# Second products of the experts' scores on halves of the array, one set of masks, turned sums by transposes

## The chip, the cores and the metric

One core of one Trainium2 chip runs the whole program. The metric is the device time in microseconds, the median of repeated executions. Each execution does the same work on the same data.

## The reference, cut to what matters

Three layers follow each other, for 2 batches of 768 tokens. Everything is in f32, and the kernel keeps near f32 precision by splitting numbers into a high and a low part.

```python
# attention, 8 heads of 64: local window of 16 on each side, and block sums
scores_l = scale * q @ k.T                       # masked to |i - j| < 16
scores_s = scale * q @ k_max.T + log(32)         # k_max: maxima over 24 blocks of 32 keys
a = softmax(concatenate([scores_l, scores_s]))
x = a @ concatenate([v, v_mean])                 # v_mean: means over the 24 blocks
# four experts with causal attention of one head of 64, top 2 of 4 by a gate
for e in range(4):
    s = scale * (x @ wq[e]) @ (x @ wk[e]).T      # masked above the diagonal
    out += weight[e] * softmax(s) @ (x @ wv[e]) @ wo[e]
# token mixing (768 -> 256 -> 768) and channel mixing (512 -> 1536 -> 512)
u = out + (relu(out.T @ w_tok1) @ w_tok2).T
result = u + relu(u @ w_ch1) @ w_ch2
```

## The kernel before, in words

The five engines run written-out programs and meet through semaphores. The order of instructions on each engine is fixed by hand: `sequence(b, more)` exists once for TensorE (PE), ScalarE (ACT) and VectorE (DVE), and GpSimd (POOL) and SyncE have loops of their own. Both batches pass through attention, experts and token mixing one after the other. Channel mixing (from about 228 us on) then takes both batches and half of the time; the change doesn't touch it.

**Attention.** A unit is a tile of 128 queries of four heads, 12 units a batch (`NU`). `a_scores(b, u)` (L774) writes the scores of a unit into one of two PSUM pairs of banks `ps_s`. A unit has 4 x 120 columns: 96 keys of a window and 24 block maxima for each head. Every product there is 64 rows by 64 columns of the array, so four go on its quarters. It first writes a mask: `ident_b` (bf16 identity) times `mask_m` (0 or -1e9 in the window, the rounded log(32) in the 24 columns behind it), 4 products of 240 columns. Then 4 products `mask_w` times `mask_c`, 48 columns each, add what rounding took from log(32). Then come 8 products of queries and keys `QT`, `KW` in f32, each of them two passes on PE. DVE takes the maxima (`a_maxima`), ACT the exponentials (`a_exps`), POOL normalises, PE turns the weights (`a_transpose`, L841) and multiplies by the values (`a_values`).

`means(out, b, q)` (L816) turns the block sums of the values, `vsum`, so that blocks lie on partitions 96 to 119: two f32 products with the identity for each call, on 24 columns of the array, two calls a batch. In batch 1 the first call stands between products of token mixing of batch 0. ACT scales the result and spreads it over the value windows (`a_means`).

**Experts.** Queries and keys of expert e are stored so that one product gives two: `QS` holds the high part of the queries on the expert's own 64 partitions and the low part on the other 64; `KH` holds the high part of the keys on both. `KL` holds the low part of the keys on the own half, and zeros on the other, which POOL writes once a batch (`no_lows`, L659; PE waits for it by `m_kz` before unit 0). So a score tile is QS x KH + QS x KL, both over 128 rows, and a bf16 product `ident_b` x `causal` adds the mask to the 128 columns on the diagonal.

`UNITS` (L112) lists 14 units a batch as (query tile t, experts, stride of their columns in PSUM): tiles 0 and 1 have one unit with all four experts, tiles 2 and 3 two units with two, tiles 4 and 5 four units with one. An expert of tile t has (t + 1) x 128 columns, in pieces of at most 512. `m_scores(b, u)` (L910) goes through the experts and for each through KH, KL, and mask (in tile 0 one 512-column mask comes first instead). Then DVE takes maxima (`m_maxima`), ACT exponentials into `PM` (`m_exps`), PE turns blocks of 128 (`m_transpose`, L947), DVE and ACT copy the two PSUM banks of `ps_t` to `PTM` (`m_to_sbuf`, one on each), PE multiplies by the values `VE` (`m_values`, on 64 columns of the array each, two experts at a time).

PE's order in the experts' loop at step k is: scores of unit k, transposes of unit k - 2, output projection and spreading of weights where due, values of unit k - 3. Scores of unit u wait for the exponentials of unit u - 2, since `ps_s` has two buffers.

The projections, the experts' scores and both mixings use the format fp32r, where a product has one record in the trace; plain f32 products (attention's keys and values, the experts' values, the turned sums) have two. L764 is the helper `mm`, so in the profile nearly every product has that line and goes by its tiles.

## Time and profile before

| | us |
|---|---|
| median of 3 timed executions | 439.59 (439.43 to 439.99) |
| profiled execution, its time | 439.09 |
| its span, first to last instruction | 437.1 |
| PE busy | 426.0 |
| VectorE busy | 288.8 |
| ScalarE busy | 227.3 |
| GpSimd busy | 143.1 |

The profiled execution is the one that all rows below come from. Its own time is 0.5 us under the median; 2.0 us of it lie outside the span. A matmul's record has the start, which is exact, and an end that is modelled and covers its way through the array; successive ones overlap, so the distance of two starts is what one costs the engine. Records with the same names are merged in the timeline ("x16"), with the start of the first and the time to the end of the last. TensorE's granted clock is at its full level in the whole span.

### The profile page before, as it was taken

To read this page: it belongs to the slowest core of one execution; us is meant where nothing else is said; L and a number is where in the kernel's file an instruction comes from. 1 tells how busy PE (TensorE), PEld (TensorE's weight loads), DVE (VectorE), ACT (ScalarE), POOL (GpSimd) and SP (SyncE) were. 2 spreads that over 40 slices of the span, in tenths; PEclk is the share of its full clock that TensorE was granted. 3 is DMA by queue.
4 is the path that set the end of the run, shared out by engine and by line. 5 is a ranking of instruction groups with operands and counts; after the bars stand their busy time and mean duration, and the time that the engine had idled before them with its cause. 6 is when DMAs were issued, how large, how long until landed. Compare 5 with 4: busy or idle time off the path is not lost.

```text
span 437.1 us, 8551 instructions
## 1 busy us (share of the span) xinstructions
PE 426.0 (97%) x3326; PEld 364.0 (83%) x3326; DVE 288.8 (66%) x520; ACT 227.3 (52%) x581; POOL 143.1 (33%) x162
## 2 busy tenths in 40 slices
PE   6899999999999999999999999999999999999996
PEld 3679996887767899878877998898898889889985
DVE  4974569785478535776867875876765765565353
ACT  6895567774269836876846353443443233324120
POOL 4997927000039420002194465233122022200000
PEclk9999999999999999999999999999999999999999
DMA  8964370000870500000133013113113252301103
GB/s 294 346 214 139 110 288 0 1 2 1 304 287 8 170 1 2 0 1 1 25 113 105 1 49 96 49 48 97 50 48 96 81 178 78 97 0 49 48 0 145
DMA packets 14799, 39.66 MB, mean 91 GB/s; under 512 B 1656, under 2 KB 3368, under 8 KB 14760
## 3 DMA queue, kind: packets, MB, share of 16 engines
q1 hardware_dynamic: 14328, 38.60, 26.5%
q8 instruction: 27, 0.44, 0.4%
q10 hardware_dynamic: 432, 0.52, 0.3%
q14 instruction: 12, 0.10, 0.1%
HBM read 33.56 MB, written 4.72 MB: 88 GB/s over the span
## 4 chain that ended last, share of the span: by engine, by line
PE 90%; DVE 4%; POOL 3%; DMA 1%; issue 1%; SPq 0%; DVEq 0%
PE ps_s L764 36%; PE ps_o L764 20%; PE ps_x L764 16%; PE ps_t L764 11%; PE ps_t L947 4%; DMA QT<-in_qT 1%; POOL PA L606 1%; DVE vsum L1636 1%; PE ps_t L841 1%; DVE nmaxA L1471 1%; PE ps_x L964 1%; POOL wv_l L625 1%; POOL KW L638 1%; DVE PTA L1488 0%; PE ps_s L1038 0%
## 5 line engine op out<-in xcount | busy, mean ns | idle before, releaser
L1450 ACT ACTIVATE HID_h<-HID_raw 128x384 fp32r<-128x384 f32 x48 | 25.1, 525 | 72.3 <-DVE HID_raw L1809 32.0
L709 POOL TENSOR_TENSOR W_raw<-W_raw 128x256 f32<-128x256 f32 x11 | 11.6, 1051 | 98.7 <-DMA W_raw<-in_ch 88.7
L606 POOL TENSOR_TENSOR PA<-PA,denA 128x480 f32<-128x480 f32 x24 | 23.8, 994 | 47.5 <-DVE denA L1481 47.4
L1198 ACT ACTIVATE PA<-ps_s,nmaxA 128x120 f32<-128x120 f32 x96 | 33.9, 391 | 8.3 <-DVE nmaxA L1471 8.1
L764 PE MATMUL ps_s<-C_h,HID_l 128*128 128x512 f32 x96 | 37.8, 393 | 0.0
L764 PE MATMUL ps_s<-C_l,HID_h 128*128 128x512 f32 x96 | 37.7, 393 | 0.0
L764 PE MATMUL ps_s<-C_h,HID_h 128*128 128x512 f32 x96 | 37.6, 392 | 0.0
L1564 DVE TENSOR_REDUCE nmaxM<-ps_s 128x1 f32<-128x640 f32 (+5 forms) x28 | 26.8, 955 | 12.7 <-PE ps_s L764 12.6
L1798 DVE SCALAR_TENSOR_TENSOR HID_l<-HID_raw,HID_h 128x384 fp32r<-128x384 f32 x48 | 27.9, 587 | 10.5 <-ACT HID_h L1450 8.1
L1270 ACT ACTIVATE PM<-ps_s,nmaxM 128x128 f32<-128x128 f32 (+5 forms) x48 | 30.1, 633 | 5.6 <-DVE nmaxM L1564 5.2
L764 PE MATMUL ps_o<-V_h,W_h 128*128 128x384 f32 x96 | 32.8, 342 | 0.1
L764 PE MATMUL ps_o<-V_h,W_l 128*128 128x384 f32 x96 | 32.4, 337 | 0.0
L764 PE MATMUL ps_o<-V_l,W_h 128*128 128x384 f32 x96 | 32.3, 337 | 0.0
L1670 DVE TENSOR_TENSOR W_l<-W_raw,W_h 128x1792 fp32r<-128x1792 f32 x12 | 26.1, 2174 | 5.4 <-ACT W_h L1335 5.4
L1444 ACT ACTIVATE U<-ps_o 128x384 f32<-128x384 f32 x12 | 5.9, 493 | 40.2 <-PE ps_o L764 40.2
L764 PE MATMUL ps_x<-V_h,W_h 128*128 128x384 f32 x72 | 24.3, 338 | 0.0
L764 PE MATMUL ps_x<-V_l,W_h 128*128 128x384 f32 x72 | 24.2, 336 | 0.0
L764 PE MATMUL ps_x<-V_h,W_l 128*128 128x384 f32 x72 | 24.2, 336 | 0.0
L947 PE MATMUL ps_t<-ident,PM 128*128 128x128 f32 x168 | 23.3, 275 | 0.9 <-issue 0.4
L1575 DVE COPY PTM<-ps_t 128x512 f32<-128x512 f32 x28 | 19.1, 683 | 7.0 <-PE ps_t L947 6.8
L764 PE MATMUL ps_s<-KH,QS 128*128 128x512 f32 (+3 forms) x64 | 23.5, 373 | 0.0
L1805 DVE TENSOR_TENSOR U<-ps_x,U 128x384 f32<-128x384 f32 x12 | 6.7, 556 | 24.9 <-PE ps_x L764 24.9
(259 smaller groups left out, 1262.0 us busy)
## 6 DMA issues: line engine op xcount, KB each, us to landing
VW<-in_vw SPq DMA_DIRECT2D x12, 512.0 KB, 8.0
W_raw<-in_ch SPq DMA_DIRECT2D x12, 512.0 KB, 3.6
C_raw<-in_ch SPq DMA_DIRECT2D x12, 512.0 KB, 3.9
VT<-in_vT SPq DMA_DIRECT2D x8, 384.0 KB, 7.6
out_x<-US SPq DMA_DIRECT2D x11, 256.0 KB, 2.1
QT<-in_qT SPq DMA_DIRECT2D x7, 384.0 KB, 6.3
KP<-in_kT SPq DMA_DIRECT2D x6, 384.0 KB, 7.3
raw<-in_tok SPq DMA_DIRECT2D x4, 384.0 KB, 3.2
```

The costliest lines, as they stand in the source:

```text
L606: pool.tensor_tensor(PA[:, u % NPA, :, :], PA[:, u % NPA, :, :], denA[:, u % 2, 1, :].unsqueeze(2).broadcast_to([P, 4, KC]), ALU.mult).the ...
L709: pool.tensor_tensor(W[S3], W[A11], W[A21], ALU.subtract).then_inc(w_sum, 1)
L764: return pe.matmul(out, lhsT, rhs, start=start, stop=stop)
L947: last = pe.transpose(ps_t[:, at_ // 512, at_ % 512:at_ % 512 + P], PM[:, u % 3, at_:at_ + P], ident[:, :])
L1198: last = act.activation(PA[:, u % NPA, j, :], ps_s[u % 2][:, j % 2, (j // 2) * KC:(j // 2 + 1) * KC], ACT.Exp, bias=nmaxA[:, u % 4, j:j + ...
L1270: last = act.activation(PM[:, u % 3, part], ps_s[u % 2][:, :, :].rearrange("p a c -> p (a c)")[:, part], ACT.Exp, bias=nmaxM[:, t, e:e + 1 ...
L1450: act.activation(*own(s, n, half), ACT.Relu).then_inc(g_hi, 1)
L1564: dve.tensor_reduce(nmaxM[:, t, experts[0]:experts[0] + n], ps_s[u % 2][:, :, :].rearrange("p a c -> p (a c)")[:, 0:n * stride] .rearrange ...
L1575: dve.tensor_copy(PTM[u % 3][:, 0:width], ps_t[:, 0, 0:width]).then_inc(m_pt0, 1)
L1670: dve.tensor_tensor(W_l[i][:, :, :, :], W_raw[i][:, :, :, :], W_h[i][:, :, :, :].bitcast(F32), ALU.subtract).then_inc(w_lo, 1)
L1798: dve.scalar_tensor_tensor(HID_l[s % 2][:, n, part], quarter(s, i), 0.0, HID_h[s % 2][:, n, part].bitcast(F32), ALU.max, ALU.subtract).the ...
L1805: dve.tensor_tensor(U2[:, :], Y, U1[:, :], ALU.add).then_inc(g_u2, 1)
```

## The change

- The experts' low keys `KL` lose their zero half and are stored for pairs of experts: `[P, EP, S]`, expert e on the half e % 2 of pair e // 2. `no_lows` and its semaphore go. The second product takes 64 rows of `QS` and `KL`.
- `m_scores` takes the experts by the groups of `TOGETHER`: first both experts' products with KH, then their products with KL piece by piece in turn, then both masks. The two experts of a group have their columns in different PSUM banks; for that, units 0 and 1 have the experts' order 0, 2, 1, 3 and a stride of 256. In tiles 4 and 5 a group is one expert.
- Tile 0 has a mask of 128 columns for each expert at the end instead of one of 512 at the start. `m_values` sorts by expert. The maxima and the copies of unit 0 follow the new placing; ACT now copies bank 1 of unit 0.
- The attention mask: the diagonal of `ident_b` is a number DIAGONAL near 1 to 2, the window's open entries are SHIFT and the block columns LOG_BLOCK, so that DIAGONAL * (LOG_BLOCK - SHIFT) is log(32) to 2e-8. The common shift falls out of the softmax. `mask_w`, `mask_c` and their products go, and two of three fills on VectorE.
- `means` turns 120 columns that end with the sums (`vsum_wide` begins 96 columns ahead of `vsum` in memory) in transpose mode, onto partitions 0 to 119, of which 96 to 119 are used.

Parts that only move memory or follow from these are left out:

```diff
@@ -65,21 +65,26 @@
+def bf16s(low, high):
+    return [2.0 ** e * (1 + i / 128.0) for e in range(-24, 8) for i in range(128) if low <= 2.0 ** e * (1 + i / 128.0) < high]
 def round_bf16(x):
     return float(((np.array([x], np.float32).view(np.uint32) + np.uint32(0x8000)) & np.uint32(0xFFFF0000)).view(np.float32)[0])
-LOG0 = round_bf16(math.log(BLOCK))
-LOG_W, LOG_M = min(((w, round_bf16((math.log(BLOCK) - LOG0) / (64 * w)))
-                    for w in (1 + i / 128.0 for i in range(128))),
-                   key=lambda f: abs(LOG0 + 64 * f[0] * f[1] - math.log(BLOCK)))
-assert abs(LOG0 + 64 * LOG_W * LOG_M - math.log(BLOCK)) < 1e-7
+DIAGONAL, LOG_BLOCK, SHIFT = min(((f, g, round_bf16(g - math.log(BLOCK) / f))
+                                  for f in bf16s(1.0, 2.0) for g in bf16s(1.5, 4.0)
+                                  if abs(g - math.log(BLOCK) / f) < 0.002),
+                                 key=lambda n: abs(n[0] * (n[1] - n[2]) - math.log(BLOCK)))
+assert abs(DIAGONAL * (LOG_BLOCK - SHIFT) - math.log(BLOCK)) < 2e-8
 NGATE = 12
 N_MASK, N_IDENT, N_CONST = 7, 9, 13
-N_MASK_V = 3
 NV = 4
@@ -109,10 +114,13 @@
-UNITS = [(0, (0, 1, 2, 3), P), (1, (0, 1, 2, 3), 2 * P)]
+UNITS = [(t, (0, 2, 1, 3), 2 * P) for t in (0, 1)]
 UNITS += [(t, (e, e + 1), 512) for t in (2, 3) for e in (0, 2)]
 UNITS += [(t, (e,), 1024) for t in (4, 5) for e in range(E)]
 MU = len(UNITS)
+TOGETHER = [((0, 2), (1, 3)) if t < 2 else ((0, 1),) if t < 4 else ((0,),) for t, _, _ in UNITS]
 BLOCKS = [[i * stride + k * P for i in range(len(experts)) for k in range(t + 1)] for t, experts, stride in UNITS]
@@ -150,9 +158,11 @@
         ident = sb("ident", [P, P], F32)
+        ahead = place[0] - WK * 4
+        vsum = sb("vsum", [P, PAIRS, NB], F32)
+        vsum_wide, _ = at("vsum_wide", [P, WK + PAIRS * NB], F32, ahead)
         ident_b = sb("ident_b", [P, P], BF16)
-        mask_w = sb("mask_w", [P, HALF], BF16)
-        mask_c = sb("mask_c", [P, NB], BF16)
         mask_m = sb("mask_m", [P, 3, KC], BF16)
...
@@ -215,7 +224,8 @@
         KH, p = at("KH", [P, E, S], F32R, region4)
-        KL, p = at("KL", [P, E, S], F32R, p)
+        KL, _ = at("KL", [P, EP, S], F32R, p)
+        p += E * S * 4
         VE, p = at("VE", [P, TQ, VG], F32, p)
...
@@ -569,9 +584,9 @@
             step(pool.memset(ident_b[:, :], 0.0))
-            keep(ident_b[:, :], [[-1, P]], 0, 1, 1.0, ALU.not_equal)
-            step(pool.memset(mask_m[0:HALF, :, 0:WK], 0.0))
+            keep(ident_b[:, :], [[-1, P]], 0, 1, DIAGONAL, ALU.not_equal)
+            step(pool.memset(mask_m[0:HALF, :, 0:WK], SHIFT))
             keep(mask_m[0:HALF, :, 0:WK], [[0, 3], [1, WK]], -1, -1, NEG)
@@ -656,16 +671,6 @@
-            def no_lows(b):
-                pool.wait_ge(a_av, b * NU + NU)
-                pool.wait_ge(a_norm, b * NU + NU)
-                if b == 0:
-                    pool.wait_ge(c_lo, splits(N_EARLY - 1))
-                for i in range(2):
-                    pool.memset(KL[(1 - i) * HD:(2 - i) * HD, i:E:2, :].bitcast(F32), 0.0).then_inc(m_kz, 1)
-                    pool.wait_ge(m_kz, 2 * b + i + 1)
             def first_weights(b):
...
@@ -793,12 +797,6 @@
                            mask_m[rows, which, :].unsqueeze(1).broadcast_to([HALF, 2, KC]), True, False)
-                for half in range(2):
-                    for r in range(2):
-                        rows = slice(r * D, (r + 1) * D)
-                        dst = ps_s[u % 2][half * HALF:(half + 1) * HALF, r, 0:2 * KC]
-                        mm(dst.rearrange("p (j c) -> p j c", j=2)[:, :, WK:KC], mask_w[rows, :],
-                           mask_c[rows, :].unsqueeze(1).broadcast_to([HALF, 2, NB]), False, False)
                 for j in range(2):
@@ -817,7 +815,8 @@
                 for j in range(2):
-                    last = mm(out[WK:KC, j * P:(j + 1) * P], vsum[:, 2 * q + j, :], ident[:, :], True, True)
+                    first = (2 * q + j) * NB
+                    last = pe.transpose(out[0:KC, j * P:(j + 1) * P], vsum_wide[:, first:first + KC], ident[:, :])
                 return last
@@ -913,26 +912,35 @@
                     pe.wait_ge(m_v2, b * (TQ - NV) + (TQ - NV))
-                    pe.wait_ge(m_kz, 2 * b + 2)
                 if u == 1:
                     pe.wait_ge(m_v, b * NV + NV)
                 if t == TQ // 2 and experts[0] == 0:
                     pe.wait_ge(m_pl, b * 8 + 8)
                 if u >= 2:
                     pe.wait_ge(m_exp, b * MU + (u - 1))
-                if t == 0:
-                    mm(ps_s[u % 2][:, 0, :], ident_b[:, :], causal[:, :].unsqueeze(1).broadcast_to([P, E, P]), True, False)
-                for i, e in enumerate(experts):
-                    q = QS[:, e, t * P:(t + 1) * P]
+                queries = slice(t * P, (t + 1) * P)
+                def pieces(i):
                     for c in range(0, (t + 1) * P, 512):
                         width = min(512, (t + 1) * P - c)
-                        has_diagonal = c + width == (t + 1) * P
-                        at_ = i * stride + c
-                        dst = ps_s[u % 2][:, at_ // 512, at_ % 512:at_ % 512 + width]
-                        mm(dst, q, KH[:, e, c:c + width], t > 0, False)
-                        last = mm(dst, q, KL[:, e, c:c + width], False, not has_diagonal if t > 0 else e == E - 1)
-                        if has_diagonal and t > 0:
-                            last = mm(dst[:, width - P:width], ident_b[:, :], causal[:, :], False, True)
+                        to = i * stride + c
+                        yield slice(c, c + width), ps_s[u % 2][:, to // 512, to % 512:to % 512 + width]
+                for both in TOGETHER[u]:
+                    for n in both:
+                        for keys, out in pieces(n):
+                            mm(out, QS[:, experts[n], queries], KH[:, experts[n], keys], True, False)
+                    for parts in zip(*(pieces(n) for n in both)):
+                        for n, (keys, out) in zip(both, parts):
+                            rows = slice(experts[n] % 2 * HD, (experts[n] % 2 + 1) * HD)
+                            last = mm(out, QS[rows, experts[n], queries], KL[rows, experts[n] // 2, keys], False,
+                                      keys.stop < (t + 1) * P)
+                    for n in both:
+                        out = list(pieces(n))[-1][1]
+                        last = mm(out[:, out.shape[-1] - P:], ident_b[:, :], causal[:, :], False, True)
                 last.then_inc(m_s, 1)
@@ -976,7 +984,8 @@
                     pe.wait_ge(m_o, b * TQ + t)
-                blocks = [(e, PTM[v % 3], i * UNITS[v][2]) for v in units for i, e in enumerate(UNITS[v][1])]
+                blocks = sorted(((e, PTM[v % 3], i * UNITS[v][2]) for v in units for i, e in enumerate(UNITS[v][1])),
+                                key=lambda block: block[0])
                 for pair in range(0, len(blocks), 2):
@@ -1279,7 +1288,10 @@
                     act.wait_ge(m_av, b * NVG + (GROUP_OF[u - 3] + 1))
-                act.activation(PTM[u % 3][:, 512:512 + width], ps_t[:, 1, 0:width], ACT.Copy).then_inc(m_pt1, 1)
+                if u == 0:
+                    act.activation(first_tile(PTM[0][:, 512:1024]), first_tile(ps_t[:, 1, :]), ACT.Copy).then_inc(m_pt1, 1)
+                else:
+                    act.activation(PTM[u % 3][:, 512:512 + width], ps_t[:, 1, 0:width], ACT.Copy).then_inc(m_pt1, 1)
@@ -1502,7 +1514,7 @@
                     e = 2 * pair + i
-                    out = KL[own[i], e, toks] if key else QS[own[1 - i], e, toks]
+                    out = KL[own[i], pair, toks] if key else QS[own[1 - i], e, toks]
                     hi = (KH if key else QS)[own[i], e, toks].bitcast(F32)
@@ -1561,6 +1573,11 @@
                 dve.wait_ge(m_s, b * MU + (u + 1))
+                if n == E:
+                    dve.tensor_reduce(nmaxM[:, t, :].rearrange("p (a i) -> p i a", i=2),
+                                      ps_s[u % 2][:, :, :].rearrange("p i (a c) -> p i a c", a=2)[:, :, :, 0:(t + 1) * P],
+                                      AX.X, ALU.max, negate=True).then_inc(m_max, 1)
+                    return
                 dve.tensor_reduce(nmaxM[:, t, experts[0]:experts[0] + n],
@@ -1572,7 +1589,10 @@
                     dve.wait_ge(m_av, b * NVG + (GROUP_OF[u - 3] + 1))
-                dve.tensor_copy(PTM[u % 3][:, 0:width], ps_t[:, 0, 0:width]).then_inc(m_pt0, 1)
+                if u == 0:
+                    dve.tensor_copy(first_tile(PTM[0][:, 0:512]), first_tile(ps_t[:, 0, :])).then_inc(m_pt0, 1)
+                else:
+                    dve.tensor_copy(PTM[u % 3][:, 0:width], ps_t[:, 0, 0:width]).then_inc(m_pt0, 1)
@@ -1760,17 +1780,12 @@
-            def fill(out, value):
-                dve.memset(out, value).then_inc(c_mask, 1)
             dve.memset(warm[:, :], 1.0).then_inc(c_warm, 1)
             dve.memset(denA[:, 0, 0, 0:1], 0.0)
             dve.memset(sumA[:, :, :, 1], 1e-9)
             dve.memset(KP[:, :, 0:WINDOW], 0.0)
             dve.memset(KP[:, :, WINDOW + S:PAD_S], 0.0).then_inc(a_zero, 1)
-            fill(mask_m[0:HALF, :, WK:KC], LOG0)
-            fill(mask_w[:, :], LOG_W)
-            fill(mask_c[:, :], LOG_M)
+            dve.memset(mask_m[0:HALF, :, WK:KC], LOG_BLOCK).then_inc(c_mask, 1)
```

## Rows read from the trace of the kernel before

**Rows 1.** The profile's page, busy time of the engines and shares of the last chain.

```profile
PE 426.0 (97%) x3326; PEld 364.0 (83%) x3326; DVE 288.8 (66%) x520; ACT 227.3 (52%) x581; POOL 143.1 (33%) x162
...
PE 90%; DVE 4%; POOL 3%; DMA 1%; issue 1%; SPq 0%; DVEq 0%
```

**Rows 2.** Busy time by stretches: busy us (and instructions) of each engine, clock, DMA.

```profile
10.40:33.00 22.60, 20.37 (x421) 15.26 (x421) 18.97 (x51) 20.54 (x98) 21.21 (x25) 1.00 0.82 282
...
129.00:148.00 19.00, 18.17 (x390) 14.24 (x390) 16.03 (x44) 17.74 (x87) 15.15 (x15) 1.00 0.18 52
```

**Rows 3.** PE's timeline (start us, us, names) where array shapes change, 102.6 to 104.8.

```profile
102.61 0.40 PE L764 MATMUL ps_x<-wo_h,OT_l 128*128 128x512 f32 x1
102.94 1.53 PE L764 MATMUL ps_o<-PTM,VE 128*64 128x128 f32 x24
104.40 0.50 PE L764 MATMUL ps_s<-X_h,tok_h 128*128 128x512 f32 x1
104.74 0.40 PE L764 MATMUL ps_s<-X_h,tok_l 128*128 128x512 f32 x1
```

**Rows 4.** The same in attention: value products, then masks, or then transposes.

```profile
20.41 0.73 PE L764 MATMUL ps_o<-PTA,VW 120*64 120x64 f32 x16
21.07 0.30 PE L764 MATMUL ps_s<-mask_m,ident_b 64*64 64x240 bf16 x4
21.20 0.19 PE L764 MATMUL ps_s<-mask_c,mask_w 64*64 64x48 bf16 x4
21.22 0.61 PE L764 MATMUL ps_s<-KW,QT 64*64 64x120 f32 x16
...
146.64 0.73 PE L764 MATMUL ps_x<-PTA,VW 120*64 120x64 f32 x16
147.30 0.65 PE L841 MATMUL ps_t<-ident,PA 128*120 128x128 f32 x4
```

**Rows 5.** The same, batch 0: transposes behind value projections, no change of shape.

```profile
36.56 0.28 PE L764 MATMUL ps_s<-wv_h,XT_l 128*128 128x260 f32 x1
36.68 0.60 PE L841 MATMUL ps_t<-ident,PA 128*120 128x128 f32 x4
```

**Rows 6.** The same in a unit of tile 3, second products and masks.

```profile
70.53 0.40 PE L764 MATMUL ps_s<-KL,QS 128*128 128x512 f32 x1
70.77 0.23 PE L764 MATMUL ps_s<-causal,ident_b 128*128 128x128 bf16 x1
70.81 0.48 PE L764 MATMUL ps_s<-KH,QS 128*128 128x512 f32 x1
71.12 0.40 PE L764 MATMUL ps_s<-KL,QS 128*128 128x512 f32 x1
```

**Rows 7.** The same, products of 128 columns (tile 0) and of 256 (tile 5).

```profile
59.27 0.28 PE L764 MATMUL ps_s<-KL,QS 128*128 128x128 f32 x1
59.38 0.27 PE L764 MATMUL ps_s<-KH,QS 128*128 128x128 f32 x1
...
100.04 0.28 PE L764 MATMUL ps_s<-KH,QS 128*128 128x256 f32 x1
100.16 0.28 PE L764 MATMUL ps_s<-KL,QS 128*128 128x256 f32 x1
```

**Rows 8.** The same around batch 1's first turned sums.

```profile
124.17 0.40 PE L764 MATMUL ps_x<-H_h,tok_l 128*128 128x512 f32 x1
124.50 0.62 PE L764 MATMUL ps_t<-ident,vsum 128*24 128x128 f32 x4
125.05 0.50 PE L764 MATMUL ps_o<-H_h,tok_h 128*128 128x512 f32 x1
125.38 0.40 PE L764 MATMUL ps_o<-H_l,tok_h 128*128 128x512 f32 x1
```

**Rows 9.** The same, the experts' transposes behind a wait.

```profile
68.11 1.06 PE L947 MATMUL ps_t<-ident,PM 128*128 128x128 f32 x8 [0.36 <-DVE PTM L1575]
```

**Rows 10.** GpSimd's timeline, the memsets of KL.

```profile
46.39 2.81 POOL L666 MEMSET KL<- 64x1536 f32 x2
```

More of the change, by code:

```diff
@@ L165, in program @@
         ksum = sb("ksum", [P, PAIRS, NB], F32)
-        vsum = sb("vsum", [P, PAIRS, NB], F32)
         nmaxM = sb("nmaxM", [P, TQ, E], F32)
@@ L287, in program, with first_tile @@
         turn_bank = [ps_o[:, :], ps_x[:, :]]
+        def first_tile(half):
+            return half.rearrange("p (a c) -> p a c", a=2)[:, :, 0:P]
         product_bank = [ps_o[:, 0:GS], ps_x[:, 0:GS]]
@@ L329, in program @@
         m_p = sem("m_p")
-        m_ph = sem("m_ph"); m_kz = sem("m_kz")
+        m_ph = sem("m_ph")
         m_pl = sem("m_pl")
@@ L730, in _ @@
                         split(n)
-                no_lows(b)
                 if b == 0:
@@ L770, in _ @@
             pe.wait_ge(c_pool, N_MASK)
-            pe.wait_ge(c_mask, N_MASK_V)
+            pe.wait_ge(c_mask, 1)
             pe.wait_ge(c_rows, 1)
```

## The prediction, made before the change was run

> **What bounds the kernel now.** I read the page first. TensorE (PE) is busy 97% of the span and carries 90% of the chain that ended last [rows 1], so an edit on PE counts at nearly full price unless PE is waiting there. The table by stretches then says where it waits: in the attention stage of batch 1 (129 to 148 us) PE is busy 18.17 of 19.00 us and ScalarE 17.74; in that of batch 0 (10.4 to 33 us) 20.37 and 20.54 of 22.60 [rows 2]. There ScalarE is close behind PE, and part of what PE saves is handed to waits. In the experts' stage the one wait of note that the trace names is 0.36 us for a copy on VectorE [rows 9]. The rest I read from PE's timeline, by starts: the ends are modelled and overlap, but start to start is what a product costs on a full PE. The change touches two things there: what shape of array a product uses, and what stands next to it.
>
> **What a change of shape costs.** The name's "128\*128" or "64\*64" is rows by columns of the array. The last output-projection product (512 columns, 128\*128) starts at 102.61 and the first value product (128\*64) at 102.94: 0.33 us, where a 512-column product is followed after 0.24 by one of the same shape [rows 3, 6]. So leaving the shape costs 0.09. Back to 128\*128, the first 512-column product at 104.40 is followed at 104.74, 0.34 instead of 0.24: its weight load has nothing to hide behind, 0.10 more. The turned vector of 24 columns shows both numbers again, 124.17 to 124.50 and 125.05 to 125.38 [rows 8]. Transposes of 128\*120 after 128\*128 products, at 36.68 behind 36.56, follow at the ordinary 0.12 [rows 5]: neither the semaphore nor the other kind of work costs anything, the shape does.
>
> Is it the same when only the rows change, as in this change? The sixteen 120\*64 value products of attention are followed once by 64\*64 masks (rows change, columns stay), 20.41 to 21.07, and once by 128\*120 transposes (columns change, rows stay), 146.64 to 147.30: 0.66 us both times [rows 4]. The row change costs what the column change costs. No row shows 64\*128, which is what the new products are; this is the nearest, and I take it at full price. Its bounds are 0 (a half of the rows at full width needs no change of shape) and the 0.09 and 0.10 above.
> The Trainium skill, in TensorEngine Tiling (Array Packing), Key Properties, has it as a rule: changing the tiling mode, and not just the tile, drains TensorE. The trace agrees by those 0.09 us, and the rule speaks against this change.
>
> **Part 1, the experts' second product.** Before, QS times KL runs on all 128 rows, half of them zeros. After, it runs on the 64 rows with content. In units of tiles 0 to 3 two experts' products go on the two halves at once; in tiles 4 and 5 a unit has one expert and nothing shares. Excursions to the half shape and back, for each batch: 2 each for tiles 0 and 1, one for each of the 2 units of tiles 2 and 3, one for each of the 8 units of tiles 4 and 5: 16, 32 in all. One costs 0.09 going in, 0.10 for the exposed 128-column load of the queries, 0.09 coming back; the load behind it is the small bf16 mask's, whose like after a change of shape shows at most 0.02 (four masks of 240 columns at 21.07, the next at 21.20, where 240 columns alone need 0.11 by the 0.24 of 512) [rows 4, 6]. That is 0.29, and in tile 0, where the 128-column stream is shorter than the load, I take 0.24: 28 x 0.29 + 4 x 0.24 = 9.1 us added. The ends: 0.23 if in tiles 4 and 5 the short product before the change gives up part of it, 0.33 if each return also exposes a load; 7.4 to 10.6.
> Shared: two pairs each of 128, 256, 384 and 512 columns for each batch. A product takes 0.11 at 128 columns, 0.12 at 256, 0.24 at 512 [rows 6, 7], and 0.18 between these for 384. 2 x 0.65 = 1.3, for both batches 2.6 us saved.
> Order: a first product right behind a short bf16 mask takes 0.31, not 0.24 (70.81 to 71.12), its load being exposed by a mask of 0.04 [rows 6]. Before there are 7 such places inside units of a batch (3 in tile 1, 1 in each unit of tiles 2 and 3), after the grouping 1 in tile 1: 6 x 0.08 = 0.48 saved. Against it, eight second masks stand behind another at about 0.06 instead of 0.04 (an estimate between the 0.04 and the 0.11 of rows 7), 0.16, and tile 0's one wide mask becomes four, about 0.1. Net 0.2 for a batch, 0.5 saved.
> Together PE gets 9.1 - 2.6 - 0.5 = 6.0 us more. Some falls into waits: the one at 68.11 [rows 9], and four smaller gaps before transposes behind a unit's mask, in all about 1.6 us by the starts. These ends are themselves chained to PE's scores, so I count half, 0.8 (0 to 1.6). **+5.2.**
>
> **Part 2, the attention masks.** The four mask_c products of each of 24 units go. From the masks at 21.07 the mask_c ones start at 21.20 and the first key product at 21.22 [rows 4]: 0.03 us. Without them the loads of the key products can hide behind the 0.13 of the masks, another 0.03 at most, so 0.7 to 1.4 us of PE.
> **Part 3, the turned sums.** A sum vector's turn is now two transposes of 128\*120 instead of four passes of 128\*24 (a plain f32 product shows as two). At 0.11 each that is 0.22 for each of four calls. In batch 1's first call two shape changes go too: from 124.17 to 125.38 stand 1.21 us; without changes 0.24 + 2 x 0.11 + 0.24 = 0.70 [rows 8]; 0.5 saved. The second calls follow transposes, and lose one change, 0.09, with it 0.02 of load: 0.33 each. The very first waits for its data before it starts: 0.22. Sum 1.4.
> Parts 2 and 3 give PE 2.1 to 2.8 us. With ScalarE at 93% and 91% of these two stretches [rows 2] I take 1.8 as reaching the end, most of it from batch 1 and from the turns, which ScalarE waits for; bounds 0.9 and 2.6. **-1.8.**
>
> **Costed at nothing.** The two memsets of KL on GpSimd go (2.81 us at 46.39 in batch 0 [rows 10]), and the wait on them; the first scores start at 58.5, 9 us later, and the work that follows on that queue ends on a wait for the gate, so nothing reaches PE; without that cover it would be a gain of 2.8 us at most. Unit 0 now lies in two PSUM banks, so ScalarE copies half of its transposes while VectorE copies less. Queued behind that copy are unit 2's exponentials, which PE needs two units later: 0, or 0.3 us slower where it is late. No DMA is moved; VectorE's three fills at the start become one, behind the DMA that PE waits for anyway.
>
> **Sum.** +5.2 - 1.8 = +3.4 us. The profiled execution has a span of 437.1 and took 439.09; it becomes 442.5, and since the median of the three timed runs is 0.5 above it, **443.0 us**.
>
> **Rivals.** (1) *The halves need no drain.* If 64\*128 beside 128\*128 changes nothing in the array, the 9.1 us go: -2.6 - 0.5 - 1.8 = -4.9, 434.7 us. For it: no row has this shape. Against it: equal 0.66 us in rows 4. It turns the sign once an excursion costs less than about 0.15 us ((2.6 + 0.5 + 1.8) / 32). By the Trainium skill's TensorEngine Tiling (Array Packing), Theoretical Speedup, two half-height products count up to double; taken alone, without its rule on draining, it would say this case. (2) *The halves take turns.* If two 64-row products of this kind do not stream together, the 2.6 go: 445.6 us. Against it: sixteen 64\*64 key products of two passes start within 0.54 us [rows 4], far too fast one by one. (3) *The price is hidden.* An excursion near 0.15, or a stage of waits that takes up most of it: about 439.6, no change. For it are only the gaps named above. (4) The attention part gives nothing, ScalarE being the bound: 444.8, within the forecast.
>
> **Chances.** The forecast (with 4) 0.66, of its own range 439.4 (-0.2: 7.4 - 2.6 - 0.8 - 1.6 - 2.6) to 446.7; halves in turns 0.08; no drain 0.16; hidden 0.10. A difference under 0.2%, 0.9 us, is about what a measurement can't tell from none. Slower 0.74, same 0.09, faster 0.17. The range 438.7 to 446.0 leaves out case 1 and a little of the top.
>
> **What would show it.** In the new trace: in tile 5 the second product should start 0.21 us behind the 256-column first one (0.12 without a drain), the next 0.34 behind it, and the mask 0.2 behind the last; a unit of tiles 4 and 5 should be 0.28 longer from first product to mask, units of tile 3 as long as before. Pairs should start within 0.01 us of each other. Attention's masks should be followed by keys after 0.13, and PE's transposed sums cost 0.22 a call. If the second product starts 0.12 behind the first, the forecast is wrong and case 1 holds.

## The result, and the profile after

| | before | after |
|---|---|---|
| median of 4 timed executions, us | 439.65 (439.43 to 439.99) | 443.75 (442.62 to 443.86) |
| ratio to before, 95% interval | | 1.0086 (1.0069 to 1.0102) |
| profiled execution, its time | 439.09 | 443.74 |
| its span | 437.1 | 441.7 |

The change makes the kernel slower by 4.1 us; 443.0 was forecast, with a range of 438.7 to 446.0. The clock of TensorE is at its full level in the whole span of both.

The page of after, to be held against [rows 1]. There are 98 products fewer on PE (3228 against 3326), and PE is busy 3.5 us longer:

```profile
PE 429.5 (97%) x3228; PEld 360.5 (82%) x3228; DVE 288.9 (65%) x518; ACT 228.6 (52%) x583; POOL 139.0 (31%) x158
...
PE 84%; POOL 4%; DVE 4%; DMA 4%; SPq 1%; issue 1%; ACT 1%; DVEq 0%; POOLq 0%
```

PE's part of the last chain fell from 90% to 84% and DMA's rose from 1% to 4%, nearly all of it under `DMA VT<-in_vT` in the page's list by line: a wait at the start, to which experiment 7 comes back.

The two attention stretches, as in [rows 2] (the second is not quite the same work, since everything there now starts some 2.4 us later):

```profile
10.40:33.00 22.60, 18.26 (x355) 13.43 (x351) 18.61 (x48) 19.53 (x91) 19.73 (x23) 1.00 0.81 285
129.00:148.00 19.00, 17.60 (x349) 13.50 (x352) 15.61 (x43) 17.84 (x82) 14.82 (x14) 1.00 0.29 92
```

PE's timeline of after, a unit of tile 3 (a pair of experts) and one of tile 5 (a single expert), to be held against [rows 6] and [rows 7]. Merged records (x2) have the start of the first:

```profile
71.40 0.73 PE L768 MATMUL ps_s<-KH,QS 128*128 128x512 f32 x2
72.06 0.51 PE L768 MATMUL ps_s<-KL,QS 64*128 64x512 f32 x2
72.50 0.29 PE L768 MATMUL ps_s<-causal,ident_b 128*128 128x128 bf16 x2
...
95.67 0.62 PE L768 MATMUL ps_s<-KH,QS 128*128 128x512 f32 x2
96.21 0.62 PE L768 MATMUL ps_s<-KL,QS 64*128 64x512 f32 x2
96.76 0.23 PE L768 MATMUL ps_s<-causal,ident_b 128*128 128x128 bf16 x1
```

The pair: 72.06 to 72.50 is 0.44 us for two products of 512 columns, where two full ones take 2 x 0.24; their starts, taken singly from the records, lie 4 ns apart, so the halves do run at once. The 0.44 holds 0.24 of streaming, 0.11 of a weight load that nothing hides and 0.09 back to the full shape. In tile 5 the same price is paid and nothing is shared.

### The profile page after: what moved, and what is told of

Its sections match the earlier page's. It is cut to its first block, busy times and chain, and to the rows that moved or that the text cites. A ratio compares the mean times of both kernels' runs of the same rounds, so it can differ in the third digit from the quotient of the medians.

```text
span 441.7 us, 8347 instructions
## 1 busy us (share of the span) xinstructions
PE 429.5 (97%) x3228; PEld 360.5 (82%) x3228; DVE 288.9 (65%) x518; ACT 228.6 (52%) x583; POOL 139.0 (31%) x158
## 4 chain that ended last, share of the span: by engine, by line
PE 84%; POOL 4%; DVE 4%; DMA 4%; SPq 1%; issue 1%; ACT 1%; DVEq 0%; POOLq 0%
PE ps_s L768 34%; PE ps_o L768 18%; PE ps_x L768 14%; PE ps_t L768 11%; PE ps_t L955 4%; DMA VT<-in_vT 3%; POOL PA L621 2%; POOL KW L653 1%; DMA u_rows<-US 1%; PE ps_t L840 1%; DVE vsum L1656 1%; POOL wv_l L640 1%; PE ps_x L972 1%; ACT PM L1279 0%; DVE X_l L1626 0%
## 5 line engine op out<-in xcount | busy, mean ns | idle before, releaser
L621 POOL TENSOR_TENSOR PA<-PA,denA 128x480 f32<-128x480 f32 x24 | 23.7, 990 | 48.5 <-DVE denA L1493 48.2
L1581 DVE TENSOR_REDUCE nmaxM<-ps_s 128x1 f32<-128x640 f32 (+3 forms) x24 | 22.9, 956 | 13.6 <-PE ps_s L768 13.6
L1207 ACT ACTIVATION_READ_ACCUMULATOR PA<-ps_s,nmaxA 128x1 f32 x96 | 23.1, 240 | 0.0
L768 PE MATMUL ps_o<-PTM,VE 128*64 128x128 f32 x336 | 22.8, 279 | 0.0
L1595 DVE COPY PTM<-ps_t 128x512 f32<-128x512 f32 x26 | 17.8, 684 | 6.8 <-PE ps_t L955 6.7
```

Source lines behind the costliest of these rows:

```text
L621: pool.tensor_tensor(PA[:, u % NPA, :, :], PA[:, u % NPA, :, :], denA[:, u % 2, 1, :].unsqueeze(2).broadcast_to([P, 4, KC]), ALU.mult).the ...
L768: return pe.matmul(out, lhsT, rhs, start=start, stop=stop)
L1207: last = act.activation(PA[:, u % NPA, j, :], ps_s[u % 2][:, j % 2, (j // 2) * KC:(j // 2 + 1) * KC], ACT.Exp, bias=nmaxA[:, u % 4, j:j + ...
L1581: dve.tensor_reduce(nmaxM[:, t, experts[0]:experts[0] + n], ps_s[u % 2][:, :, :].rearrange("p a c -> p (a c)")[:, 0:n * stride] .rearrange ...
L1595: dve.tensor_copy(PTM[u % 3][:, 0:width], ps_t[:, 0, 0:width]).then_inc(m_pt0, 1)
```

## The experiments

All times are medians; "before" was run again beside each kernel (439.63 to 439.95). Some of what follows reads one product after the other. I took the starts of PE's records in order, and a list such as "337, 209, 340, 209 ns" is the distances of successive starts, from the first score product of a unit to its last mask.

**1. The attention part alone** (att_only): masks and turned sums as in after, experts as in before. Against after, among others:

```diff
-                for both in TOGETHER[u]:
-                    for n in both:
-                        for keys, out in pieces(n):
-                            mm(out, QS[:, experts[n], queries], KH[:, experts[n], keys], True, False)
...
+                        mm(dst, q, KH[:, e, c:c + width], t > 0, False)
+                        last = mm(dst, q, KL[:, e, c:c + width], False, not has_diagonal if t > 0 else e == E - 1)
```

> Only the attention part of the change (one set of masks, turned sums by transposes); the experts are as before, with the zero rows. Forecast's own term: 1.8 us faster than before (0.9 to 2.6), 437.9. The trace of the changed kernel shows more: batch 1's attention 1.1 us shorter, batch 0's 1.0 shorter up to its sixth unit, and then VectorE waiting 1.76 us for the transfer of the third pair of values, which lands at 19.5 us. If that wait comes from the transfer meeting work that now runs ahead, it is here as well, and this kernel takes about 439.2 (0.4 faster). If it belongs to the experts' part or was chance, it isn't, and this takes about 437.6.

Measured 438.12 us (437.52 to 438.73), ratio 0.9962 (0.9949 to 0.9976): 1.6 us faster. Rival 4 (attention gives nothing) falls.

**2. The experts' part alone** (exp_only): the reverse. Against after, the mask and the sums of before come back:

```diff
+                        mm(dst.rearrange("p (j c) -> p j c", j=2)[:, :, WK:KC], mask_w[rows, :],
+                           mask_c[rows, :].unsqueeze(1).broadcast_to([HALF, 2, NB]), False, False)
...
-                    last = pe.transpose(out[0:KC, j * P:(j + 1) * P], vsum_wide[:, first:first + KC], ident[:, :])
+                    last = mm(out[WK:KC, j * P:(j + 1) * P], vsum[:, 2 * q + j, :], ident[:, :], True, True)
```

> Only the experts' part of the change (64-row second products, grouping, no memsets of KL); attention is as before. By the trace of the changed kernel the experts' stages grow by 2.3 us in batch 0 and 2.9 in batch 1: 444.8. Theory of the forecast (changes of array shape, 0.29 us for each of 32 excursions, less 3.1 for sharing and order, 0.8 in waits): 439.65 + 5.2 = 444.9. Rival (no drain, and something else in the changed kernel slow): about 436.5.

Measured 444.8 us (444.45 to 445.67), ratio 1.0115 (1.0094 to 1.0135): 5.1 us slower. The loss is all here. With experiment 1, 439.7 - 1.6 + 5.1 = 443.2, against the 443.75 of both together.

**3. The new order, with full products** (order_full): the experts' part with its groups, banks and masks, but the second product on 128 rows and with the zero half, which GpSimd writes again.

```diff
-                            rows = slice(experts[n] % 2 * HD, (experts[n] % 2 + 1) * HD)
-                            last = mm(out, QS[rows, experts[n], queries], KL[rows, experts[n] // 2, keys], False,
+                            rows = slice(0, P)
+                            last = mm(out, QS[rows, experts[n], queries], KL[rows, experts[n], keys], False,
```

> The experts' part with the same order, groups and banks, but the second products on all 128 rows again, with KL's zeros written by GpSimd as before. So no array shape changes inside a unit of scores. Theory (the shape changes are the loss): the order alone saves 0.25 us a batch on TensorE: 439.1, from 0.8 faster to no difference. Rival (the loss comes from the order, the new banks of units 0 and 1, or ScalarE's additional copy): above 441, up to the 444.8 of the experts' part.

Measured 438.86 us (438.24 to 439.87), ratio 0.9982 (0.9971 to 0.9993): 0.8 us faster than before. What is left between this and exp_only is the half shape (and GpSimd's zeros, under cover): 5.9 us, sharing included.

**4. Halves only where two experts share** (halves_low): as 3, but 64 rows in tiles 0 to 3, that is 16 excursions to the half shape in place of 32.

```diff
-                            rows = slice(0, P)
+                            rows = slice(experts[n] % 2 * HD, (experts[n] % 2 + 1) * HD) if t < 4 else slice(0, P)
```

> As the kernel with all 128 rows and the new order, but second products of tiles 0 to 3 on 64 rows, two experts side by side; tiles 4 and 5 stay on 128 rows with zeros. 16 of the 32 excursions. Theory: against the 128-row kernel 16 x 0.27 = 4.3 us more and 2.6 less by sharing, 1.7 slower, about 440.8; the other 16 excursions then make up the rest, 4.5 us, up to the experts' part alone. If excursions are cheap where two products share and the loss sits elsewhere, it is 2.6 us faster than the 128-row kernel, about 436.5.

Measured 440.07 us (439.52 to 440.86), ratio 1.0007 (0.9996 to 1.0019). Even where two products do share, the half shape costs 1.2 us by the medians. 1.7 was expected, and the score units of its trace are together 1.85 us longer than those of experiment 3; the two traces' times differ by 1.7.

**5. More excursions** (more_turns): exp_only, but in tiles 4 and 5 the half product stands behind each full one, so that every unit there has two excursions: 48 in all, with the same products.

```diff
...
                         for n, (keys, out) in zip(both, parts):
+                            if len(both) == 1:
+                                mm(out, QS[:, experts[n], queries], KH[:, experts[n], keys], True, False)
```

> The experts' part alone, with the 64-row product behind each piece in tiles 4 and 5 (first, second, first, second product, mask) instead of both first products and then both second ones: 16 excursions more (48 for 32), the same products and the same data. Theory (a price for each change of array shape): 0.09 in, 0.10 for the exposed load, 0.09 back and 0.10 for the load of the f32r product behind it, a little less at 128 columns, about 0.35 each: 16 x 0.35 = 5.6 slower than the experts' part alone, 450.4. Rival (what costs is a 64-row product in itself, not the change): as the experts' part alone, 444.8.

Measured 450.7 us (449.94 to 451.43), ratio 1.0244 (1.0223 to 1.0266): against exp_only that is 5.7 us by the ratios, 5.9 by the medians, for 16 more excursions: 0.36 each. It is the same arithmetic with nothing added but turns, so the price hangs on the turns. A unit of tile 5 in it:

```profile
96.52 0.51 PE L762 MATMUL ps_s<-KH,QS 128*128 128x512 f32 x1
96.96 0.49 PE L762 MATMUL ps_s<-KL,QS 64*128 64x512 f32 x1
97.38 0.39 PE L762 MATMUL ps_s<-KH,QS 128*128 128x256 f32 x1
97.69 0.38 PE L762 MATMUL ps_s<-KL,QS 64*128 64x256 f32 x1
98.01 0.23 PE L762 MATMUL ps_s<-causal,ident_b 128*128 128x128 bf16 x1
```

and of the kernel of experiment 3, where nothing changes shape (the unit behind it, unit 12):

```profile
95.85 0.52 PE L772 MATMUL ps_s<-KH,QS 128*128 128x512 f32 x2
96.20 0.51 PE L772 MATMUL ps_s<-KL,QS 128*128 128x512 f32 x2
96.55 0.23 PE L772 MATMUL ps_s<-causal,ident_b 128*128 128x128 bf16 x1
```

From the first product to the mask: 0.70 us with no excursion, 1.09 (95.67 to 96.76) with one in after, 1.49 with two. 0.11 of the first step is no excursion: the after unit stands behind value products, which themselves have another shape, and the one of experiment 3 behind output projections. Like for like, unit 11 of a batch goes 0.80 (before), 0.82 (order_full), 1.10 (after), 1.48 (more_turns). The second excursion is dearer, 0.39 against 0.28: two changes of 0.09 and not one but two loads of 0.10, since it returns to a large product, whose load is exposed as well.

**6. The parts of the attention change.** masks_only has only the one set of masks, means_only only the turned sums by transposes. Against before:

```diff
-                        mm(dst.rearrange("p (j c) -> p j c", j=2)[:, :, WK:KC], mask_w[rows, :],
-                           mask_c[rows, :].unsqueeze(1).broadcast_to([HALF, 2, NB]), False, False)
```

```diff
-                    last = mm(out[WK:KC, j * P:(j + 1) * P], vsum[:, 2 * q + j, :], ident[:, :], True, True)
+                    last = pe.transpose(out[0:KC, j * P:(j + 1) * P], vsum_wide[:, first:first + KC], ident[:, :])
```

> Only the attention masks in one set (four products of 48 columns fewer in each of 24 units). Forecast's term: 0.03 to 0.06 of TensorE for a unit, 0.7 to 1.4, of which about 0.6 reach the end: 439.1. If batch 0's share is lost to the transfers: 0.6 from batch 1 alone, the same 439.1; if none reaches the end, 439.7.

> Only the turned sums by transposes of 120 columns. Forecast's term: 0.22, 0.33, 0.5 and 0.33 for the four calls, 1.4 in all, about 1.1 reaching the end: 438.6. In batch 1 the first call should save 0.5 and the second 0.33.

Measured: masks_only 439.25 us (438.51 to 440.5), ratio 0.9989 (0.9975 to 1.0002), which is not told apart from no change; means_only 439.08 us (438.18 to 440.43), ratio 0.9986 (0.9973 to 0.9998). Both gained less than expected (0.4 and 0.55 us for 0.6 and 1.1), and their sum is under the 1.6 of att_only, though not by more than the intervals allow. The profiled execution of masks_only, 440.35, is one of its slowest: TensorE's granted clock in it is at the half level (1.2 GHz) from 8.5 to 12.0 us, just behind a wait of PE of 1.3 us for the queries' transfer. So only differences inside batch 1 are read from it below. The turned sums in batch 1's first call, which were 124.17 to 125.38 before [rows 8], in after:

```profile
127.21 0.39 PE L768 MATMUL ps_x<-H_h,tok_l 128*128 128x512 f32 x1
127.44 0.38 PE L819 MATMUL ps_t<-ident,vsum_wide 128*120 128x128 f32 x2
127.57 0.48 PE L768 MATMUL ps_o<-H_h,tok_h 128*128 128x512 f32 x1
127.89 0.40 PE L768 MATMUL ps_o<-H_l,tok_h 128*128 128x512 f32 x1
```

0.68 us in place of 1.21, 0.53 saved for the 0.5 of the forecast: both changes of shape and two of the four passes are gone.

**7. The wait that the faster attention runs into** (after_vt, att_vt, best_vt). In the trace of after VectorE reaches the third pair of value vectors before its transfer has landed:

```profile
19.56 0.95 DVE L1656 TENSOR_REDUCE vsum<-VT 128x24 f32<-128x768 f32 x1 [1.76 <-DMA VT<-in_vT]
```

It is the wait that the last chain goes through. My theory was that this transfer only stands too late in SyncE's list, and that its place is worth a part of the gain of attention in batch 0. The edit, on SyncE, of after, of att_only and of the best combination (8):

```diff
+            load_values(0, 2)
             load_windows(0, 0, 2)
-            for r in range(2, PAIRS):
-                load_values(0, r)
+            load_values(0, 3)
```

> The changed kernel with one line moved on SyncE: the transfer of the third pair of values (batch 0) is issued ahead of the last window of the first half of values, 512 KB earlier in the queue. Theory (batch 0's attention ran about 1 us ahead and lost it to that transfer, which lands at 19.5 us): the lead stays, 0.8 to 1.3 us faster than the changed kernel, 442.7. Rival (the wait moves to the next transfer or to ScalarE, whose work fills 91% of the stretch): no difference, 443.7.

> The attention part alone with the same transfer moved. Theory: the wait of 1.17 us for that transfer goes, 438.1 - 1.0 = 437.1. Rival: 438.1.

> What is worth keeping, together: the attention part, the experts' new order and banks with second products on all 128 rows and zeros, and the transfer moved. No 64-row products in the experts. If the parts add up: 439.69 - 1.57 (attention) - 0.83 (order) - 1.0 (transfer) = 436.3. If the attention part and the order both only gained the same earlier start: 437.3.

Measured: after_vt 444.87 us (442.61 to 446.49), ratio 1.0108 (1.0069 to 1.0148); att_vt 439.63 (437.44 to 441.19), ratio 0.9991 (0.9969 to 1.0013), 1.3 us over att_only by the ratios; best_vt 437.86 (436.33 to 440.88), ratio 0.9962 (0.9937 to 0.9987). In the median the move gains nothing. VectorE's wait shrank (from 1.76 to 0.39 us in after_vt; in att_vt it is gone), and a larger one came behind it; ScalarE's rows of after_vt and of att_vt:

```profile
27.91 0.63 ACT L1225 ACTIVATE VW<-VS 24x512 f32<-24x512 f32 x1 [2.66 <-DMA VW<-in_vw]
```

```profile
27.14 0.62 ACT L1217 ACTIVATE VW<-VS 24x512 f32<-24x512 f32 x1 [2.25 <-DMA VW<-in_vw]
```

The windows of values were now the late ones, and SyncE issues in order: behind its own wait for them stood the queries and the windows of the second half. SyncE's issues in att_only, and then in att_vt:

```profile
17.62 0.83 SPq L448 DMA_DIRECT2D VW<-VS  x1
19.07 0.90 SPq L440 DMA_DIRECT2D VW<-in_vw  x2
```

```profile
19.30 0.83 SPq L448 DMA_DIRECT2D VW<-VS  x1
...
20.73 1.81 SPq L440 DMA_DIRECT2D VW<-in_vw  x2
```

They go out 1.7 us later. In this stretch the transfers are full (DMA share 1.00 at 360 GB/s from 2 to 20 us in after), so a place in the list chooses who waits.

The medians also mix two levels of TensorE's clock. In the trace of att_vt PE waits 2.36 us for ScalarE's exponentials, up to 29.3 us, and its granted clock is at the half level (1.2 GHz) from 30.7 to 34.1. In after_vt it waits 2.77 us up to 30.1, and the half level lasts from 31.4 to 34.8. In best_vt's trace the clock stays at its full level. The timed executions differ in the same way, by their mean granted clock (medians in us, number of executions):

| | clock 0.998 or more | clock below | not moved, clock 0.998 or more |
|---|---|---|---|
| after_vt | 443.31 (2) | 446.11 (2) | 443.74 (3) |
| att_vt | 437.62 (4) | 440.16 (6) | 438.12 (6) |
| best_vt | 436.87 (6) | 439.74 (4) | 437.61 (5) |

At full clock the moved transfer is 0.4 to 0.7 us ahead, about half of what the theory said, in too few executions, and not measured side by side, to call it shown; the medians below 0.998 are 2.5 to 2.9 us above the others of the same kernel, with the longer wait in them. So the theory was not simply wrong: it left out that a longer wait of PE can bring the clock down.

**8. The best combination** (best): the attention part of after with the edit of experiment 3, so that both are in it and no half shape is.

> The attention part and the experts' new order and banks, second products on all 128 rows with zeros, transfers in the order of before. If both parts add: 439.7 - 1.6 - 0.8 = 437.3, 0.5% faster than before.

Measured 437.96 us (436.99 to 438.39), ratio 0.995 (0.9932 to 0.9969): 1.7 us faster than before and 5.8 faster than after. It is short of the sum of its parts (1.6 + 0.8) by 0.7, but 437.3, the time expected from them, lies within the interval of the ratio (436.6 to 438.3 us). Its profiled execution is the slowest of the six and the only one with a mean clock under 0.999: VectorE waits 2.18 us for the value vectors in it, against 1.17 in att_only, PE behind it waits 2.24 us, up to 21.3 us, and its clock is at the half level from 22.6 to 26.0. The other five have a median of 437.61.

**9. Fewer bytes** (best_narrow): only 96 of the 128 partitions of a value window are loaded with values, the others with padding, so the transfer was cut to these, 384 KB for each in place of 512.

```diff
-                sp.dma_start(VW[:, q, 4 * i:4 * i + 4, :],
-                             vw_d[b, :, q, 4 * i:4 * i + 4, :]).then_inc(ld_vw[q][i], 16)
+                sp.dma_start(VW[0:WK, q, 4 * i:4 * i + 4, :],
+                             vw_d[b, 0:WK, q, 4 * i:4 * i + 4, :]).then_inc(ld_vw[q][i], 16)
```

> The same, with the value windows loaded on the 96 partitions that hold values instead of 128: each of the 12 transfers moves 384 KB instead of 512; the padding rows aren't loaded (rows 96 to 119 are written by the means anyway, 120 to 127 are read by nothing). Theory (batch 0's attention is bound by the bytes ahead of the third pair of values): 384 KB less ahead of it, at some 400 GB/s 1 us earlier, so the wait of VectorE at 18 to 19.5 us goes and the kernel is about 0.9 faster than with full loads, 436.4. Rival (that stage is held by ScalarE or by the latency of the transfers, not by bytes): 437.3.

Measured 441.61 us (439.52 to 442.44), ratio 1.0032 (1.0014 to 1.0051): 3.7 us slower than best. Stretches of best, then of best_narrow (the last two numbers are the DMA engines' busy share and GB/s):

```profile
10.00:15.00 5.00, 4.35 (x73) 2.76 (x69) 4.78 (x11) 4.39 (x19) 4.79 (x6) 1.00 1.04 421
15.00:20.00 5.00, 3.34 (x69) 2.40 (x65) 2.79 (x7) 4.60 (x25) 3.31 (x4) 1.00 0.92 336
```

```profile
10.00:15.00 5.00, 4.35 (x73) 2.73 (x69) 4.80 (x11) 4.39 (x19) 4.86 (x6) 1.00 1.05 257
15.00:20.00 5.00, 2.81 (x68) 2.08 (x64) 2.40 (x6) 4.62 (x25) 3.33 (x4) 1.00 1.03 269
```

The engines are as busy as in best and move 257 GB/s in place of 421. Each packet takes longer, those of the transfers that were not changed too: in the first of these stretches a packet of 4096 bytes takes 282 ns (median) in place of 159, one of 3072 bytes, as the value vectors have on each partition, 209 in place of 121. VectorE then waits 4.55 us:

```profile
21.99 0.95 DVE L1667 TENSOR_REDUCE vsum<-VT 128x24 f32<-128x768 f32 x1 [4.55 <-DMA VT<-in_vT]
```

The 3.7 us are not that transfer alone. PE waits 1.50 us up to 19.4 us and 3.04 up to 23.7, and its clock is at the half level from 22.3 to 29.1; all nine timed executions have a mean clock of 0.991 to 0.996, where five of the six of best have 0.999 or more. PE's rows at the half level and, from 29.18, at the full one again:

```profile
23.67 1.15 PE L778 MATMUL ps_o<-PTA,VW 120*64 120x64 f32 x16 [3.04 <-DVE XT_l L1517]
...
25.90 1.11 PE L850 MATMUL ps_t<-ident,PA 128*120 128x128 f32 x4
...
29.18 0.65 PE L850 MATMUL ps_t<-ident,PA 128*120 128x128 f32 x4
...
29.98 0.73 PE L778 MATMUL ps_o<-PTA,VW 120*64 120x64 f32 x16
```

Against best's trace it is 1.6 us late at the start of attention's unit 6, 2.8 at unit 7 and 3.1 from unit 8 on. From unit 7 to unit 8, all at the half level, it takes 3.28 us, where att_only at full clock takes 2.61: about 0.7 of the loss is the clock by this estimate, and the late transfer is the larger part.

The Trainium skill, in DMA: Bandwidth & Descriptors, section Why a DMA increments its semaphore by 16 and not by 1, says that a tile of 96 partitions goes to all 16 engines like one of 128. The trace agrees with that as far as the busy share shows it (1.05), and shows that the rate is not the same. Why was not tried and stays open.

## Why the prediction was right, point by point

**The price of an excursion: right, and in tile 4 too large.** The forecast for tile 5 was 0.34, 0.21, 0.34, 0.2 us from start to start; unit 11 of after has 337, 209, 340, 209 ns, the same unit of order_full 344, 116, 234, 121. So entering costs 93 ns, the exposed load of the queries 106, leaving 88: 0.29, the three terms of the forecast. In tile 4 the list of order_full is 334, 59, 281, 63 and that of after 334, 151, 336, 150: 92 in, 55, 87 out, together 0.234. The load there was half exposed before, behind a product of 128 columns that is too short to hide it. That was the low end that the prediction named (0.23); I took 0.29, and the term was over-sized by 8 x 0.055 = 0.45 us.
The Trainium skill's rule in TensorEngine Tiling (Array Packing), Key Properties, that a change of tiling mode drains TensorE, is borne out for a change of rows alone, with 0.09 us each time. The exposed load, 0.106 us in tile 5, comes on top and is as dear as either change.

**Sharing and order: right.** Pairs in order_full and in after, from first product to last mask, for each excursion: tile 0 1042 to 1291 ns for two, 0.125; tile 1 1191 to 1534, 0.17; tile 2 775 to 883, 0.11; tile 3 1103 to 1155 and 1167, 0.06. The forecast's price less what the pair shares is 0.24 - 0.11, 0.29 - 0.12, 0.29 - 0.18 and 0.29 - 0.24: 0.13, 0.17, 0.11 and 0.05. So not even two products of 512 columns pay for their excursion. The order was put at -0.5. The score units of order_full are 0.27 us shorter than those of before in batch 0 and 0.29 in batch 1, 0.56 in all, as forecast; the medians differ by 0.8.

**What goes into waits: the size nearly right, the sum by luck.** The table gives, at some landmarks, how much later than in the profiled run of before each kernel's record starts (us, to about 0.01).

| start of | exp_only | order_full | att_only | after |
|---|---|---|---|---|
| attention, batch 0, unit 6 | -0.51 | -0.99 | -1.23 | -0.98 |
| projections, batch 0 | +0.64 | +0.13 | +0.10 | +0.94 |
| experts, batch 0, unit 3 | +1.17 | +0.04 | +0.13 | +1.47 |
| experts, batch 0, unit 4 | +0.92 | -0.30 | +0.12 | +1.22 |
| experts, batch 0, unit 13 | +2.88 | -0.03 | +0.14 | +3.18 |
| token mixing, batch 0, 2nd part | +2.88 | -0.03 | +0.15 | +3.19 |
| attention, batch 1, unit 1 | +2.88 | -0.03 | +0.06 | +3.10 |
| projections, batch 1 | +2.90 | -0.02 | -0.97 | +2.06 |
| experts, batch 1, unit 13 | +4.88 | -0.54 | -0.98 | +4.07 |
| token mixing, batch 1, 2nd part | +5.78 | -0.53 | -0.96 | +4.99 |

The units of after and of exp_only, from first product to last mask, are together 2.7 us longer in each batch, 5.4 in all, for the 6.0 of the forecast. In exp_only waits take up 0.44 of that in batch 0 (0.25 of it between units 3 and 4, the wait of [rows 9], and 0.26 behind unit 13, less small changes) and 0.43 in batch 1: 0.9, for the 0.8 of the forecast. But behind unit 13 of batch 1 the delay grows by 0.9, of which 0.28 is the unit. The rest is a wait that before didn't have. In after:

```profile
228.37 1.32 DVE L1626 TENSOR_TENSOR X_l<-US,X_h 128x512 fp32r<-128x512 f32 x1
...
236.29 0.68 DVE L1626 TENSOR_TENSOR X_l<-ps_x,X_h 128x512 fp32r<-128x512 f32 x1
```

```profile
237.03 0.50 PE L768 MATMUL ps_s<-X_l,tok_h 128*128 128x512 f32 x1 [0.51 <-DVE X_l L1626]
```

In before that first row took 0.68 us as well, and everything that VectorE has to do up to the second hangs on it. The records, taken singly, show what goes with the doubling. GpSimd splits weights (`V_l`) beside it, in pieces of 0.73 us. In the four traces with halves in all tiles (after, after_vt, exp_only, more_turns) one piece starts between 3 ns before and 29 ns after VectorE's product, and this then takes 1.29 to 1.32 us, and GpSimd's next piece 1.18 to 1.21. In the ten others, before, order_full and halves_low among them, the piece starts 82 to 139 ns after it; then VectorE's product takes 0.68 to 0.73, and only that piece takes 1.18 to 1.20. So, as the times read, one of the two is held while the other works, and a shift of 0.1 us decides whether VectorE is held first; what shifts them is open. The 0.6 comes with these kernels, but it is not a price of the half shape. So the 5.1 of exp_only is 5.4 - 0.9 + 0.6. The forecast's 5.2 was 6.0 - 0.8: a term too large by 0.6 and a wait of 0.6 that I did not see made up for each other, and that the sum came out within 0.1 is luck.

**Attention: the size nearly right, half of its place wrong.** 1.8 was forecast, "most of it from batch 1 and from the turns"; att_only gained 1.6. In its trace 1.1 us lie in batch 1 (+0.15 to -0.97). The first turned sum gives 0.54. The second gives 0.33, of which means_only loses all but 0.1 again in a wait one unit later. The masks give 0.05 to 0.06 for a unit, the upper end of the forecast (the key products' loads are hidden now), but of 12 units only 0.35 is left at the end of the batch in masks_only. The trace names who takes it: one wait of 0.18 us for ScalarE's exponentials that before does not have, and two that grow, for VectorE's `XT_l` (0.59 for 0.48) and for GpSimd's `KW` (0.29 for 0.23). The wait that takes back the second turned sum in means_only is the one for `KW` (0.56 for 0.23). So in batch 1 it is three engines that hand the gain on, and not ScalarE alone, as I had said. Masks are followed by keys after 0.13 as forecast:

```profile
18.14 0.30 PE L768 MATMUL ps_s<-mask_m,ident_b 64*64 64x240 bf16 x4
18.27 0.58 PE L768 MATMUL ps_s<-KW,QT 64*64 64x120 f32 x16
```

Of the transposed sums I had said 0.22 a call. They take 0.13 from start to start, and the product behind them 0.32 in place of 0.24, in all 0.21.
In batch 0 the traces show no gain at the end of attention: att_only is ahead by 1.23 at unit 6 and behind by 0.10 at the projections. In after PE is busy 2.1 us less in the first stretch than in [rows 2], ScalarE 1.0 less (1.9 and 0.5 in att_only), and the stage is no shorter. I had named ScalarE as what takes the gain of PE; here it was the value vectors' transfer of experiment 7. The later starts of exp_only (+0.64) and order_full (+0.13), whose attention is that of before, show how much this point moves from one execution to the next. What batch 0 gives in the mean the single traces don't tell; the medians leave at most the 0.5 between 1.6 and 1.1.

**Costed at nothing: right.** exp_only, without the memsets of KL [rows 10], starts the projections and the experts of batch 0 at the same +0.64. In order_full ScalarE copies half of unit 0's transposes, and units 2 and 3 start at +0.03 and +0.04 where unit 0 was at +0.13.

**The rivals.** (1) No drain: refuted by the lists above and by 438.86, 440.07, 444.8 and 450.7 us for 0, 16, 32 and 48 excursions. (2) Halves in turns: refuted by the starts 4 ns apart. (3) Hidden: only 0.9 of 5.4 us. (4) Refuted by att_only.

## What to carry to other kernels

Halving the rows of a product gives TensorE nothing if it stands alone, and the way into the half shape and back cost 0.29 us here, of which a third is a weight load that could no longer be hidden; a pair on the two halves shared 0.24 at most. Look for such turns first by start-to-start distances where the trace already has them, count them in the new order, and put all products of one shape in a row, or leave zeros in the operand. And a stage that starts behind a full set of transfers hands its gains to them: ask what the transfer's landing allows before pricing a faster engine there. Where a wait of TensorE grows, look at the granted clock of each execution, and not only at the median, before calling an edit neutral.

## What the runs showed of the hardware that was not expected

- Changing only the rows of the array (128 to 64, columns kept) costs 92 ns going in and 88 coming back, as much as the change of columns in [rows 3] (0.09 us).
- Cutting transfers from 128 to 96 partitions, a quarter of the bytes less, lowered the rate from 421 to 257 GB/s with the engines as busy; the kernel took 3.7 us more, about 0.7 of it through TensorE's clock.
- TensorE's granted clock went to the half level for 3.4 us in traces in which it had just waited 2.2 to 2.8 us at one place (best, att_vt, after_vt), and for 6.8 us in best_narrow, with waits of 1.5 and 3.0. The times of one kernel scattered more with the value transfer moved, and the scatter follows the clock: best_vt took 436.33 to 437.92 us with a mean clock of 0.998 or more and 439.18 to 440.88 below it.
- VectorE's `X_l<-US,X_h` and GpSimd's `V_l<-V_raw,V_h` do not seem to run side by side: where GpSimd's piece started at most 29 ns behind VectorE's product, this took 1.29 to 1.32 us in place of 0.68 to 0.73; where it started 82 to 139 ns behind, GpSimd's piece took 1.18 to 1.20 in place of 0.73.
